# Fused attention and two MLPs: the first tile's layer 1 with its last block made for all 512 tokens at once, and the second product of probabilities and values issued one half block sooner

## The chip, the cores and the metric

The kernel runs on one core of one Trainium2 chip. The metric is the device time of the launch in microseconds. The kernel before takes 1432.98 us, the median of 3 runs (1432.86 to 1433.89).

## The reference

Attention over pooled keys and values, followed by two feed-forward layers, all in float32:

```
k_p = k.reshape(B, H, 72, 8, 64).mean(3);  v_p likewise        # 576 positions pooled by 8
attn = softmax(q @ k_p^T / 8);  x = attn @ v_p                 # B = H = 8, S = 576, D = 64
x = x as (4608 tokens, 512)
h = max(x @ w1, x @ w2, x @ w3);  x2 = h @ w_mid               # 512 -> 768 -> 512
y = x2 @ w_in;  out = (y - tanh(y)) @ w_out                    # 512 -> 2048 -> 512
```

## The kernel before, in words

**Tiling.** The 4608 tokens are 9 tiles of 512 (`TB`). Float32 products are made from operands split into a high and a low part, with three matmuls for each product (high by high, high by low, low by high; `split_passes`, line 611). Layer 1 of a tile is 6 blocks `m` of 128 hidden features. A block needs three products (w1, w2, w3; `NW`), each of 4 chunks `c` of the inputs and so of 12 matmuls: 36 matmuls in all. Attention comes in steps of 128 tokens: "score" (products of q and keys), "exp", "norm" (sums of rows and their inverse), "turn" (normalise, then transpose), and "attend", the product of probabilities and values, which gives `x`. The attends are listed in `ATTENDS` (line 84): two of 256 tokens for tile 0, then one of 512 for each tile.

**Order.** `make_order` (line 106) writes one list, `ORDER`. PE, DVE, ACT and SP each walk this list and do their share of every entry, so an entry's place sets the order on every queue at once. Within an entry the engines meet through semaphores. The entries are these:
- `("l1", t, m, lo, hi)` is block m of tile t for the tokens lo to hi. On PE it is `layer1` (line 672). On ACT it is `copy_first` (line 854), which copies the first product out of PSUM. On DVE it is `take_max` (line 1101): L1108 takes the maximum with the second product, L1113 that with the third.
- `("h1", ...)` splits this maximum: ACT makes the high part (L866), DVE the low part (L1119), which raises `h1_ready`.
- `("score", n)` is L625 on PE, then L1057 and L1061 on DVE and L847 on ACT. `norm` is L1073, L1076 and L1079, `turn` is L1087 and L1092, all on DVE.
- `("attend", n)` is L665 on PE, L852 on ACT and L1098 on DVE. The last of these raises `x_ready`.
- `("high", i)` splits a piece of weights on ACT (L837). For `w123` blocks 2 to 5 and both halves of `w_mid` POOL makes the low part (L590).
- `kred` and `vred` pool the keys and values of a batch on DVE (L1040, L1047). They stand in a list `waiting`, and each `fill()` puts the next group of it into the order.
- `("l2", t, c)` is a 512-token block of the middle layer, 18 matmuls on PE (L696), three for each m. For c = 0 PE waits before each m until `h1` of that block is ready. DVE takes it apart in `x2_sums` (line 1122).

**Tile 0.** Each of the 6 blocks is made twice: for tokens 0 to 255 as soon as the first attend has given them, and for tokens 256 to 511 after the second attend. There are thus 12 entries of 36 matmuls of 256 columns. Score 4 and 5 follow the first block of the second half, score 6 and 7 the fourth.

**PSUM.** Banks 0 to 3 are shared out by a counter (lines 183 to 190): each l1 entry takes the next three banks in turn, each l2 entry the next one, modulo 4. PE's `open_bank` (line 630) waits until the bank's use before has been drained. There are 60 l1 entries and 36 l2 entries, 216 uses in all. The last four are the l2 blocks of the last tile in the order c = 0, 2, 1, 3; they fall on banks 0, 1, 2, 3. The last of them is drained in DVE's step 2 at L1144, the one before it at L1142.

**The seam to the last layers.** After step 2 of the 72 steps of the large layer, PE runs `first_project`, the first products with `w_out`, which accumulate in banks 0 to 3 for the four groups j of 128 tokens. `project` (line 706) waits, for m = 0, until bank j has been drained of all its uses:

```python
                    for js in ((0, 1), (2, 3)):
                        for c in range(2):
                            project(c, js)
...
                    if m == 0:
                        if t == 0:
                            pe.wait_ge(drained[j], BANK_USES[j])
```

DVE's step 2 has, between the two halves of its own work, the two lines

```python
                    x2_sums(("l2", NT - 1, C_ORDER[2]))
                    x2_sums(("l2", NT - 1, C_ORDER[3]))
```

Of the kernel before, what the change touches and what calls it, by code (L numbers as in the profile page):

```python
# [22 lines left out]
MC1 = FF1 // P  # L23
# [4 lines left out]
TB = 512  # L28
NT = TOKENS // TB
SUB = TB // P  # L30
HALF = TB // 2
# [26 lines left out]
UNITS = STEPS2 * KHALF  # L58
# [28 lines left out]
def products_until(t, pair=PAIRS - 1):  # L87

    return PAIRS * (t + 1) + pair + 1
# [16 lines left out]
def make_order():  # L106

    o = [("kred", 0, p) for p in range(PAIRS)] + [
        ("warm", 14), ("score", 0), ("score", 1), ("exp", 0), ("exp", 1), ("warm", 14), ("pool_v",), ("warm", 6), ("norm", 0),
        ("high", 0), ("norm", 1), ("turn", 1), ("turn", 0), ("low", 0), ("attend", 0), ("high", 1), ("low", 1), ("high", 2)]  # L110
    waiting = []

    def then(*entries):
        for e in entries:
            o.append(e)
            if e[0] == "score" and e[1] != 3:
                o.append(("exp", e[1]))
            if e[0] == "score" and e[1] in LAST_STEP[:-2]:
                b = LAST_STEP.index(e[1]) + 2
                waiting.extend([[("kred", b, 0), ("kred", b, 1)], [("kred", b, 2), ("kred", b, 3)]])  # L120
            if e[0] == "attend" and 2 <= e[1] < B:
                waiting.extend([[("vred", e[1], 0), ("vred", e[1], 1)], [("vred", e[1], 2)]])

    def fill():
        if waiting:
            o.extend(waiting.pop(0))

    def l1(t, m, lo, hi):
        then(("l1", t, m, lo, hi), ("h1", t, m, lo, hi))

    def split(*pieces):
        return [(part, i) for i in pieces for part in ("high", "low")]

    waiting.extend([[("kred", 1, 0), ("kred", 1, 1)], [("kred", 1, 2), ("kred", 1, 3)],
                    [("vred", 1, 0)], [("vred", 1, 1)], [("vred", 1, 2)]])
    after_l1 = [[("high", 3), ("score", 2), ("score", 3), ("norm", 2), ("turn", 2)], [("high", 4), ("norm", 3)],
                [("high", 5), ("turn", 3)], [("high", 6)], [("attend", 1)], [("high", 7)]]
    for m in range(MC1):
        if m == 1:
            then(("l1", 0, m, 0, HALF), ("exp", 3), ("h1", 0, m, 0, HALF))  # L140
        else:
            l1(0, m, 0, HALF)
        then(*after_l1[m])
        if m > 1:
            fill()

    for t in range(NT):
        a = 4 * t + 4
        after_l1 = [[("score", a), ("score", a + 1), ("norm", a), ("turn", a)], [("norm", a + 1), ("turn", a + 1)], [],
                    [("score", a + 2), ("score", a + 3), ("norm", a + 2), ("turn", a + 2)],  # L150
                    [("norm", a + 3), ("turn", a + 3)], []]
        if t == 0:
            after_l1[4:] = [[], [("norm", a + 3), ("turn", a + 3)]]
        if t == NT - 1:
            after_l1 = [[("load", ("out", 0))], [("load", ("out", 1)), ("load_w", 0)], split(8) + [("load_w", 1)], split(9),
                        [("load_x2",)], []]
        for m in range(MC1):
            l1(t, m, HALF if t == 0 else 0, TB)
            if t > 0 and MC1 * (t - 1) + m < 2 * UNITS:
                then(("w_split", (MC1 * (t - 1) + m) // 2, m % 2))  # L160
            then(*after_l1[m])
            if m in (2, 4, 5):
                fill()
        if t == NT - 1:
            break
        for i, c in enumerate(C_ORDER):
            then(("l2", t, c))
            if i % 2:
                then(("x2_split", t, i // 2))
            if i == 1:  # L170
                then(("attend", t + 2))
            if i % 2:
                fill()

    then(("l2", NT - 1, C_ORDER[0]), ("step", 0), ("x2_part", NT - 1, C_ORDER[1]), ("step", 1),
         ("step", 2), ("first_project",))
    assert not waiting
    return o


ORDER = make_order()

USES, BANK_USES, _at = {}, [0] * 4, 0
for _e in ORDER + [("l2", NT - 1, c) for c in C_ORDER[1:]]:
    if _e[0] in ("l1", "l2"):
        USES[_e] = []
        for _i in range(NW if _e[0] == "l1" else 1):
            USES[_e].append((_at % 4, BANK_USES[_at % 4]))
            BANK_USES[_at % 4] += 1
            _at += 1  # L190
L1_NUMBER = {e: i for i, e in enumerate(e for e in ORDER if e[0] == "l1")}
for _kind, _count in (("score", STEPS), ("exp", STEPS), ("norm", STEPS), ("turn", STEPS), ("attend", len(ATTENDS)), ("step", EARLY)):
    assert sorted(e[1] for e in ORDER if e[0] == _kind) == list(range(_count))
assert [e[1] for e in ORDER if e[0] == "high"] == list(range(len(PIECES) - len(LATE)))
# [2 lines left out]
def fused_attention_mlps(nc, q, k, v_0, v, w123_in, w_mid, w_in, w_out, out):  # L197
# [5 lines left out]
    with ExitStack() as ctx:  # L203
        def sem(name):
            return ctx.enter_context(nc.semaphore(name))
# [124 lines left out]
        h1_ready = sem("h1_ready")  # L330
# [46 lines left out]
        def wait_piece(eng, kind, n):  # L377
            if (kind, n) in LOW_ON_POOL:
                eng.wait_ge(low_by_pool, LOW_ON_POOL.index((kind, n)) + 1)
            else:  # L380
                eng.wait_ge(low_by_dve, LOW_ON_DVE.index((kind, n)) + 1)
# [228 lines left out]
        def _(pe):  # L610
            def split_passes():
                return ((0, 0), (0, 1), (1, 0))
# [17 lines left out]
            def open_bank(entry, n=0):  # L630
                bank, before = USES[entry][n]
                if before > 0:
                    pe.wait_ge(drained[bank], before)
                return bank
# [37 lines left out]
            def layer1(entry):  # L672
                _, t, m, lo, hi = entry
                if t == 0 and lo == 0:
                    wait_piece(pe, "w123", m)
                for n in range(NW):
                    bank = open_bank(entry, n)
                    for c in range(KC1):
                        if m == 0 and n == 0:
                            pe.wait_ge(x_ready, c + 1 if hi == HALF else products_until(t, c))  # L680
                        for ws, xs in split_passes():
                            mm = pe.matmul(psum[:, bank, 0:hi - lo], w123[:, m, ws, n, c, :],  # L682
                                           x[:, xs, c, lo:hi],
                                           start=(c == 0 and ws + xs == 0), stop=(c == KC1 - 1 and ws == 1))
                    mm.then_inc(filled[bank], 1)

            def layer2(entry, ms=range(MC1)):
                _, t, c = entry
                if t == 0 and c == 0:
                    wait_piece(pe, "mid", 1)  # L690
                bank = open_bank(entry)
                for m in ms:
                    if c == 0:
                        pe.wait_ge(h1_ready, L1_NUMBER[("l1", t, m, HALF if t == 0 else 0, TB)] + 1)
                    for ws, xs in split_passes():
                        mm = pe.matmul(psum[:, bank, :], w_mid_s[:, ws, m, c * P:(c + 1) * P], h1[:, xs, m, :],  # L696
                                       start=(m == 0 and ws + xs == 0), stop=(m == MC1 - 1 and ws == 1))
                if ms[-1] == MC1 - 1:
                    mm.then_inc(filled[bank], 1)
# [133 lines left out]
        def _(act):  # L833
# [20 lines left out]
            def copy_first(entry):  # L854
                i = L1_NUMBER[entry]
                _, t, m, lo, hi = entry
                bank = wait_filled(act, entry)
                nc.scalar.activation(first_copy[:, i % 2, 0:hi - lo], psum[:, bank, 0:hi - lo], ACT.Copy)\
                    .then_inc(drained[bank], 1)

            def h1_high(entry):
                i = L1_NUMBER[entry]
                _, t, m, lo, hi = entry
                bank, before = USES[entry][2]
                act.wait_ge(drained[bank], before + 1)
                nc.scalar.activation(h1[:, 0, m, lo:hi], best[:, i % 2, 0:hi - lo], ACT.Copy).then_inc(h1_hi_ready, 1)  # L866
# [162 lines left out]
        def _(dve):  # L1029
# [71 lines left out]
            def take_max(entry):  # L1101
                i = L1_NUMBER[entry]
                _, t, m, lo, hi = entry
# [11 lines left out]
            def h1_low(entry):  # L1115
                i = L1_NUMBER[entry]
                _, t, m, lo, hi = entry
                dve.wait_ge(h1_hi_ready, i + 1)
                nc.vector.tensor_tensor(h1[:, 1, m, lo:hi], best[:, i % 2, 0:hi - lo], as_f32(h1[:, 0, m, lo:hi]),  # L1119
                                        ALU.subtract).then_inc(h1_ready, 1)  # L1120
# [204 lines left out]
```

## Time and profile before

| | |
|---|---|
| Median of 3 runs | 1432.98 us |
| Profiled execution | 1433.14 us, its span 1431.3 us |
| PE busy | 1421.7 us, 99% of the span |
| DVE busy | 1015.7 us, 71% |
| ACT busy | 661.2 us, 46% |
| POOL busy | 97.0 us, 7% |
| DMA | 269.74 MB, mean 188 GB/s |
| Mean granted TensorE clock | 1.000 |

The span runs from the first to the last instruction. The 1.84 us by which the execution is longer lie around it. PE's busy time counts modelled ends of pipelined matmuls, so 99% says that it seldom waits, and not that it is at its peak. Matmuls and weight loads are each recorded with a line of the kernel; the helpers' lines are those named above.

### The profile page before, as it was taken

To read this page: it belongs to the slowest core of one execution; us is meant where nothing else is said; L and a number is where in the kernel's file an instruction comes from. 1 tells how busy PE (TensorE), PEld (TensorE's weight loads), DVE (VectorE), ACT (ScalarE), POOL (GpSimd) and SP (SyncE) were. 2 spreads that over 40 slices of the span, in tenths; PEclk is the share of its full clock that TensorE was granted. 3 is DMA by queue.
4 is the path that set the end of the run, shared out by engine and by line. 5 is a ranking of instruction groups with operands and counts; after the bars stand their busy time and mean duration, and the time that the engine had idled before them with its cause. 6 is when DMAs were issued, how large, how long until landed. Compare 5 with 4: busy or idle time off the path is not lost.

```text
span 1431.3 us, 26330 instructions
## 1 busy us (share of the span) xinstructions
PE 1421.7 (99%) x10788; PEld 1236.2 (86%) x10788; DVE 1015.7 (71%) x1764; ACT 661.2 (46%) x1291; POOL 97.0 (7%) x141
## 2 busy tenths in 40 slices
PE   8999999999999999999999999999999999999998
PEld 7988888888888878788889999899999999999897
DVE  7876666666666655534887777877777777777787
ACT  4322222222222221223666666666666666666655
POOL 3402121212121100000000000000000000000000
PEclk9999999999999999999999999999999999999999
DMA  9254444443534211155976665666756666575641
GB/s 345 82 184 139 165 140 165 142 163 125 185 121 157 86 71 41 66 185 194 371 258 243 228 249 210 233 235 220 259 213 247 217 226 252 204 274 201 212 177 52
DMA packets 81335, 269.74 MB, mean 188 GB/s; under 512 B 7168, under 2 KB 21504, under 8 KB 69568
## 3 DMA queue, kind: packets, MB, share of 16 engines
q1 hardware_dynamic: 81216, 268.07, 52.1%
q8 instruction: 85, 1.39, 0.4%
q14 instruction: 34, 0.28, 0.1%
HBM read 210.89 MB, written 57.15 MB: 187 GB/s over the span
## 4 chain that ended last, share of the span: by engine, by line
PE 98%; DMA 1%; DVE 1%; ACT 0%; issue 0%; SPq 0%; ACTq 0%
PE psum L682 31%; PE psum L722 27%; PE psum L744 25%; PE psum L696 10%; PE psum L625 2%; PE psum L665 2%; DMA v_first<-in_v 0%; DMA k_first<-in_k 0%; PE psum L817 0%; ACT g L897 0%; PE psum L644 0%; DVE w L1052 0%; DVE poly L1175 0%; DVE g L1154 0%; ACT w L837 0%
## 5 line engine op out<-in xcount | busy, mean ns | idle before, releaser
L682 PE MATMUL psum<-x,w 128*128 128x512 f32 (+1 forms) x2160 | 451.6, 369 | 2.5 <-issue 1.2
L682 PEld LDWEIGHTS psum<-x,w 128*128 128x128 f32 x2160 | 375.5, 188 | 72.9 <-issue 2.1
L722 PE MATMUL psum<-w_out_s,g 128*128 128x512 f32 x1668 | 391.7, 390 | 0.1
L722 PEld LDWEIGHTS psum<-w_out_s,g 128*128 128x128 f32 x1668 | 308.6, 188 | 61.6 <-DVE g L1154 0.5
L744 PEld LDWEIGHTS psum<-x_even,ring 128*128 128x128 f32 x1680 | 208.2, 192 | 3.4
L744 PE MATMUL psum<-x_even,ring 128*128 128x256 f32 x1680 | 210.3, 283 | 0.0
L913 ACT ACTIVATE copies<-psum 128x256 f32<-128x256 f32 x288 | 108.0, 381 | 219.3 <-PE psum L744 217.9
L744 PEld LDWEIGHTS psum<-x_odd,ring 128*128 128x128 f32 x1344 | 166.3, 192 | 2.5
L744 PE MATMUL psum<-x_odd,ring 128*128 128x256 f32 x1344 | 168.2, 283 | 0.0
L866 ACT ACTIVATE h<-best 128x512 fp32r<-128x512 f32 (+1 forms) x60 | 35.3, 589 | 276.7 <-DVE best L1113 276.7
L696 PE MATMUL psum<-h,w_mid_s 128*128 128x512 f32 x648 | 151.7, 391 | 0.0
L696 PEld LDWEIGHTS psum<-h,w_mid_s 128*128 128x128 f32 x648 | 120.7, 188 | 28.6 <-issue 3.4
L1154 DVE TENSOR_TENSOR g<-poly,g 128x512 fp32r<-128x512 f32 x140 | 96.5, 689 | 52.0 <-ACT g L897 51.9
L1159 DVE SCALAR_TENSOR_TENSOR poly<-poly,u_sq 128x512 f32<-128x512 f32 x144 | 98.6, 685 | 21.7 <-ACT poly L910 21.6
L897 ACT ACTIVATE g<-poly 128x512 fp32r<-128x512 f32 x140 | 89.0, 636 | 52.6 <-DVE poly L1175 46.8
L910 ACT ACTIVATE poly<-u_sq,shift_col 128x512 f32<-128x512 f32 x144 | 103.3, 718 | 2.4
L1175 DVE COPY_PREDICATED poly<-is_big,h 128x512 f32<-128x512 uint8 x136 | 100.6, 740 | 2.4
L1169 DVE SCALAR_TENSOR_TENSOR poly<-poly,h 128x512 f32<-128x512 f32 x144 | 98.6, 684 | 0.0
L1113 DVE TENSOR_TENSOR best<-psum,best 128x512 f32<-128x512 f32 (+1 forms) x60 | 38.3, 639 | 83.8 <-PE psum L682 83.0
L1171 DVE TENSOR_TENSOR h<-h,tanh_h 128x512 f32<-128x512 f32 x136 | 93.2, 685 | 0.0
L901 ACT ACTIVATE u_sq<-h 128x512 f32<-128x512 f32 x144 | 90.4, 628 | 3.5 <-DVE h L1191 1.3
L904 ACT ACTIVATE tanh_h<-h 128x512 f32<-128x512 f32 x136 | 84.3, 620 | 0.0
(84 smaller groups left out, 1026.2 us busy)
## 6 DMA issues: line engine op xcount, KB each, us to landing
ring<-w_scratch SPq DMA_DIRECT2D x72, 1024.0 KB, 7.3
ring<-w_scratch SPq DMA_DIRECT2D x72, 768.0 KB, 4.4
x_scratch<-x_stage SPq DMA_DIRECT2D x18, 1024.0 KB, 4.2
x_odd<-x_scratch SPq DMA_DIRECT2D x28, 512.0 KB, 5.6
x_even<-x_scratch SPq DMA_DIRECT2D x28, 512.0 KB, 5.5
x_scratch<-x_stage SPq DMA_DIRECT2D x18, 768.0 KB, 3.3
w_scratch<-w_stage SPq DMA_DIRECT2D x32, 384.0 KB, 2.6
v_raw<-in_v SPq DMA_DIRECT2D x21, 512.0 KB, 4.4
```

What stands on the lines that cost most here:

```text
L682: mm = pe.matmul(psum[:, bank, 0:hi - lo], w123[:, m, ws, n, c, :], x[:, xs, c, lo:hi], start=(c == 0 and ws + xs == 0), stop=(c == KC1 - ...
L696: mm = pe.matmul(psum[:, bank, :], w_mid_s[:, ws, m, c * P:(c + 1) * P], h1[:, xs, m, :], start=(m == 0 and ws + xs == 0), stop=(m == MC1 ...
L722: mm = pe.matmul(psum[:, j, :], g_of(c)[:, gs, j * P:(j + 1) * P], w_out_s[:, row_of(c), ws, :], start=(m == 0 and gs + ws == 0), stop=(m ...
L744: mm = pe.matmul(psum[:, bank, 0:HALF], ring[:, p % 2, n, j, ws], x2[t % 2][:, j, X_OF[n], xs], start=(fresh and j + ws + xs == 0), stop=( ...
L901: nc.scalar.activation(u_sq[:, e], h2[:, s % 2, e], ACT.Square).then_inc(sq_done, 1)
L910: nc.scalar.activation(poly[:, into], u_sq[:, e], ACT.Square, bias=shift_col[:, 0:1]).then_inc(sq_done, 1)
L913: nc.scalar.activation(copies[:, n], psum[:, main_banks(s)[1 if n == 3 else 0], 0:HALF], ACT.Copy)\
L1154: nc.vector.tensor_tensor(g_of(c)[:, 1, :], poly[:, e], as_f32(g_of(c)[:, 0, :]), ALU.subtract).then_inc(g_ready, 1)
L1159: nc.vector.scalar_tensor_tensor(out=poly[:, into], in0=poly[:, into], scalar=OFFSET, in1=u_sq[:, e], op0=ALU.add, op1=ALU.mult).then_inc( ...
L1169: nc.vector.scalar_tensor_tensor(out=poly[:, into], in0=poly[:, into], scalar=C2, in1=h, op0=ALU.mult, op1=ALU.mult)
L1171: nc.vector.tensor_tensor(h, h, gelu_of(s)[0][:, e], ALU.subtract).then_inc(dve_step, 1)
L1175: nc.vector.copy_predicated(poly[:, into], gelu_of(s)[1][:, e], h2[:, s % 2, e]).then_inc(h_drained, 1)
```

## The change

The first half of tile 0 (tokens 0 to 255) now has blocks 0 to 4 alone. Turn 3 comes after block 1 and not after block 2. The second attend comes after block 3 and not after block 4. Block 5 is then made once, for all 512 tokens, and waits for `x` of the second attend. After it come score 4 and 5 with norm 4 and turn 4, and one `fill()`. Blocks 0 to 4 of the second half follow, with score 6 and 7 after block 2, and `fill()` after blocks 1, 3 and 4. Tile 0 has 11 l1 entries where it had 12. The loop over tiles skips layer 1 for tile 0. `L1_LAST` holds the last entry of each block, for the middle layer's waits. The later tiles' entries are unchanged.

```diff
--- before.py
+++ after.py
@@ -133,9 +133,10 @@
 
     waiting.extend([[("kred", 1, 0), ("kred", 1, 1)], [("kred", 1, 2), ("kred", 1, 3)],
                     [("vred", 1, 0)], [("vred", 1, 1)], [("vred", 1, 2)]])
-    after_l1 = [[("high", 3), ("score", 2), ("score", 3), ("norm", 2), ("turn", 2)], [("high", 4), ("norm", 3)],
-                [("high", 5), ("turn", 3)], [("high", 6)], [("attend", 1)], [("high", 7)]]
-    for m in range(MC1):
+    after_l1 = [[("high", 3), ("score", 2), ("score", 3), ("norm", 2), ("turn", 2)], [("high", 4), ("norm", 3), ("turn", 3)],
+                [("high", 5)], [("high", 6), ("attend", 1)], [("high", 7)]]
+
+    for m in range(MC1 - 1):
         if m == 1:
             then(("l1", 0, m, 0, HALF), ("exp", 3), ("h1", 0, m, 0, HALF))
         else:
@@ -143,20 +144,27 @@
         then(*after_l1[m])
         if m > 1:
             fill()
+    l1(0, MC1 - 1, 0, TB)
+    then(("score", 4), ("score", 5), ("norm", 4), ("turn", 4))
+    fill()
+    after_l1 = [[("norm", 5), ("turn", 5)], [], [("score", 6), ("score", 7), ("norm", 6), ("turn", 6)], [], [("norm", 7), ("turn", 7)]]
+    for m in range(MC1 - 1):
+        l1(0, m, HALF, TB)
+        then(*after_l1[m])
+        if m in (1, 3, 4):
+            fill()
 
     for t in range(NT):
         a = 4 * t + 4
         after_l1 = [[("score", a), ("score", a + 1), ("norm", a), ("turn", a)], [("norm", a + 1), ("turn", a + 1)], [],
                     [("score", a + 2), ("score", a + 3), ("norm", a + 2), ("turn", a + 2)],
                     [("norm", a + 3), ("turn", a + 3)], []]
-        if t == 0:
-            after_l1[4:] = [[], [("norm", a + 3), ("turn", a + 3)]]
         if t == NT - 1:
             after_l1 = [[("load", ("out", 0))], [("load", ("out", 1)), ("load_w", 0)], split(8) + [("load_w", 1)], split(9),
                         [("load_x2",)], []]
-        for m in range(MC1):
-            l1(t, m, HALF if t == 0 else 0, TB)
-            if t > 0 and MC1 * (t - 1) + m < 2 * UNITS:
+        for m in range(MC1 if t > 0 else 0):
+            l1(t, m, 0, TB)
+            if MC1 * (t - 1) + m < 2 * UNITS:
                 then(("w_split", (MC1 * (t - 1) + m) // 2, m % 2))
             then(*after_l1[m])
             if m in (2, 4, 5):
@@ -189,6 +197,8 @@
             BANK_USES[_at % 4] += 1
             _at += 1
 L1_NUMBER = {e: i for i, e in enumerate(e for e in ORDER if e[0] == "l1")}
+
+L1_LAST = {e[1:3]: e for e in ORDER if e[0] == "l1"}
 for _kind, _count in (("score", STEPS), ("exp", STEPS), ("norm", STEPS), ("turn", STEPS), ("attend", len(ATTENDS)), ("step", EARLY)):
     assert sorted(e[1] for e in ORDER if e[0] == _kind) == list(range(_count))
 assert [e[1] for e in ORDER if e[0] == "high"] == list(range(len(PIECES) - len(LATE)))
@@ -676,7 +686,7 @@
                 for n in range(NW):
                     bank = open_bank(entry, n)
                     for c in range(KC1):
-                        if m == 0 and n == 0:
+                        if n == 0 and (m == 0 or (t, m, lo, hi) == (0, MC1 - 1, 0, TB)):
                             pe.wait_ge(x_ready, c + 1 if hi == HALF else products_until(t, c))
                         for ws, xs in split_passes():
                             mm = pe.matmul(psum[:, bank, 0:hi - lo], w123[:, m, ws, n, c, :],
@@ -691,7 +701,7 @@
                 bank = open_bank(entry)
                 for m in ms:
                     if c == 0:
-                        pe.wait_ge(h1_ready, L1_NUMBER[("l1", t, m, HALF if t == 0 else 0, TB)] + 1)
+                        pe.wait_ge(h1_ready, L1_NUMBER[L1_LAST[t, m]] + 1)
                     for ws, xs in split_passes():
                         mm = pe.matmul(psum[:, bank, :], w_mid_s[:, ws, m, c * P:(c + 1) * P], h1[:, xs, m, :],
                                        start=(m == 0 and ws + xs == 0), stop=(m == MC1 - 1 and ws == 1))
```

## Rows read from the trace of the kernel before

Times are in us from the span's start unless marked ns. A row of an engine in order of time has its start, its length, the engine, line and operation, output and input with their shapes, and in brackets how long the engine was idle before it and who ended that.

**Rows 1.** The page: the chain that ended last, by engine, and the granted clock in 40 slices.
```profile
PEclk9999999999999999999999999999999999999999
...
PE 98%; DMA 1%; DVE 1%; ACT 0%; issue 0%; SPq 0%; ACTq 0%
```

**Rows 2.** The chain in order of time, around tile 0: start us, us, what.
```profile
30.37 14.29 PE psum L682 x117
...
46.14 8.82 PE psum L682 x72
54.97 1.64 PE psum L625 x103
...
80.53 8.20 PE psum L696 x36
...
100.11 8.21 PE psum L682 x36
```

**Rows 3.** DVE in order of time, tile 1: start us, us, engine, line, operation, idle before.
```profile
108.36 0.69 DVE L1113 TENSOR_TENSOR best<-psum,best 128x512 f32<-128x512 f32 x1 [1.56 <-PE psum L682]
...
110.35 0.75 DVE L1057 TENSOR_REDUCE row_max<-psum 128x8 f32<-128x576 f32 x1
```

**Rows 4.** DVE in order of time, tile 0's second half.
```profile
56.99 0.75 DVE L1057 TENSOR_REDUCE row_max<-psum 128x8 f32<-128x576 f32 x1
...
62.97 0.38 DVE L1108 TENSOR_TENSOR best<-psum,first_copy 128x256 f32<-128x256 f32 x1
...
64.70 0.75 DVE L1073 TENSOR_REDUCE row_sum<-probs 128x8 f32<-128x576 f32 x1
...
67.62 0.39 DVE L1108 TENSOR_TENSOR best<-psum,first_copy 128x256 f32<-128x256 f32 x1
...
69.36 1.21 DVE L1047 TENSOR_REDUCE v_pooled<-v_raw 128x128 f32<-128x1024 f32 x1
70.49 0.41 DVE L1108 TENSOR_TENSOR best<-psum,first_copy 128x256 f32<-128x256 f32 x1
...
72.26 0.75 DVE L1057 TENSOR_REDUCE row_max<-psum 128x8 f32<-128x576 f32 x1
...
78.24 0.38 DVE L1108 TENSOR_TENSOR best<-psum,first_copy 128x256 f32<-128x256 f32 x1
...
79.98 1.41 DVE L1040 TENSOR_REDUCE k_pooled<-k_raw 128x72 f32<-128x576 f32 x2
81.30 0.42 DVE L1108 TENSOR_TENSOR best<-psum,first_copy 128x256 f32<-128x256 f32 x1
...
82.73 0.42 DVE L1119 TENSOR_TENSOR h<-best,h 128x256 fp32r<-128x256 f32 x1 [0.48 <-ACT h L866]
```

**Rows 5.** DVE in order of time, tile 0's first half.
```profile
35.05 0.20 DVE L1079 RECIPROCAL row_inv<-row_eps 128x8 f32<-128x8 f32 x1
...
37.91 1.85 DVE L1087 TENSOR_TENSOR probs<-probs,row_inv 128x576 f32<-128x576 f32 x1
...
47.56 1.41 DVE L1098 TENSOR_TENSOR x<-psum,x 128x256 fp32r<-128x256 f32 x4
```

**Rows 6.** Line L1087: count, duration ns min/median/max, first and last start.
```profile
L1087 DVE TENSOR_TENSOR probs<-probs,row_inv x35: 757/759/1848, 13.9 to 580.7; 128x576 f32<-128x576 f32 x35
```

**Rows 7.** POOL in order of time, the low parts of blocks 4 and 5.
```profile
35.15 8.29 POOL L590 TENSOR_TENSOR w<-w_raw,w 128x512 fp32r<-128x512 f32 x6 [4.82 <-ACT w L837]
```

**Rows 8.** PE in order of time, the first products with w_out.
```profile
684.76 5.63 PE L722 MATMUL psum<-w_out_s,early_g 128*128 128x512 f32 x24
```

**Rows 9.** DVE in order of time, beside it.
```profile
686.75 0.42 DVE L1144 TENSOR_TENSOR x_stage_raw<-psum,x_stage_raw 128x256 f32<-128x256 f32 x1
```

**Rows 10.** The chain at PE's first wait for x: start us, us, what.
```profile
19.36 0.14 issue
```

**Rows 11.** PE in order of time, two stretches of warm-up matmuls of one shape.
```profile
1.10 5.40 PE L704 MATMUL psum<-ones 128*128 128x128 f32 x28 [1.10 <-POOL ones L570]
...
9.11 3.39 PE L704 MATMUL psum<-ones 128*128 128x128 f32 x28
```

## The prediction, made before the kernel was built

> **What bounds the kernel now.** I read the chain that ended last first: 98% of it is PE, and the granted clock is full in every slice [rows 1]. A change pays only if it shortens PE's own work, and costs whatever it makes PE wait. Next I read the chain in order of time around tile 0, because it gives the price of a block of each width and shows no gap between 30.37 us and the middle layer [rows 2]. Since PE is gapless there, what matters is how close the other engines are behind it. So I read DVE in order of time: in the second half of tile 0 it runs from 56.99 to 83.15 us with hardly a pause [rows 4]. Last I went to a place far away, where PE starts on w_out, because the bank of every later PSUM use hangs on the number of l1 entries [rows 8, 9].
>
> **PE's own work.** Removed: two passes over block 5 of 36 matmuls each at 256 columns; added: one of 36 at 512 columns. Two half blocks took 8.82 us, the whole block in tile 1 took 8.21 us [rows 2]. The gain is 0.61 us. The rest of PE's work (scores, attend, the ten other half blocks) only changes places.
> The isolated gap of the Trainium skill ("TensorE: Matmul & The Clock Gate", Back-to-back issue gap) has a fixed part of 2.5 ns for each matmul, which would make this an estimated 36 x 2.5 ns = 0.09 us. The two rows differ by 17 ns for each matmul saved, and they decide.
>
> **The second attend, one half block sooner.** Old PE times first: 117 matmuls from 30.37 took 14.29 us, 0.122 each, and the attend stood at 44.66, with 1.48 us to 46.14 [rows 2]. With 36 matmuls fewer ahead of it, it stands at 40.26 and ends at 41.74. It needs turn 3, which DVE now does right after norm 3, from about 35.3 us [rows 5]. The normalising multiply usually takes 0.76 us [rows 6]. Old turn 3 took 1.85 [rows 5] while POOL was at work [rows 7], and POOL starts on block 4 at 35.15, so I take 1.85. The transpose is then over at about 38.1, two microseconds ahead of the attend. Behind turn 3 on DVE waits `take_max` of block 2, now at 38.1 to 38.5. PE wants its bank for the third product of block 3 at 30.37 + 69 x 0.122 = 38.8. That is free by 0.3 us; a second delay of 1.1 us by POOL would turn it into a stall of 0.8 us, and the multiply at its usual 0.76 us leaves 1.4 us. ACT's split of the weights of block 5 follows `h1` of block 2 and so moves to about 39.4 to 40.9; POOL's three subtractions (half of 8.29 us, [rows 7]) end at about 45.0. PE needs them at 46.15, so the margin is 1.1 us. The split of `x` on DVE took 1.41 us [rows 5] and has PE's half block 4 (4.41 us) as its cover, as it had half block 5 before; ahead of it stands a weight split of ACT, and I get the last `x` at 46.1 to 46.4, where the first product needs only chunk 0 and chunk 3 comes 2 us later. Cost of this part: nothing, bounds 0 and +1 us. On SP, the loads of queries, keys and values keep their partners, and all these are used more than 10 us after issue: nothing. The wait for `x` inserted in `layer1` has behind it on PE block 5, and nothing else that could run.
>
> **DVE behind the whole block.** New times on PE: half block 4 ends at 46.15, block 5 at 54.36, the scores (1.64 us) at 56.00, which is 0.61 sooner than before. In tile 1 the whole block ended at 100.11 + 8.21 = 108.32 [rows 2] and DVE reached the scores at 110.35 [rows 3], 2.03 us later. So DVE starts on score 4 at 56.39. From there every entry is queued without a pause. The durations are differences of starts in [rows 4]: score 4 and 5 with norm and turn 4, 5.98 (56.99 to 62.97); vred, 1.13 (69.36 to 70.49), **which now stands here**, while before it stood ahead of the scores, where DVE had time; maximum and split of half block 0, 1.73; norm 5 and turn 5, 2.92; half block 1, 1.74; the last vred, 1.13; half block 2, 1.77; score 6 and 7 with norm and turn 6, 5.98; half block 3, 1.74; two kred, 1.32; half block 4 to the end of its low part, 1.85 (81.30 to 82.73 + 0.42). The sum is 27.29 us, and the last low part is ready at 83.68; with 0.14 us from DVE to PE [rows 10] PE can go on at 83.82.
> PE without stalls would begin the middle layer at 80.53 - 0.61 = 79.92. Before, the last block to be ready was block 5, which PE needs after 15 matmuls. Now it is block 4, needed after 12: 12 x 8.20/36 = 2.73 us, at 82.65 [rows 2]. By ends of matmuls the wait is 1.17 us. By starts, which lie 0.16 sooner, it is 1.33. I take **+1.25 us**. It will show in pieces, since DVE also frees banks late: I expect the first and largest (0.7 us) at the third product of half block 1, which waits for L1108 of half block 0. Smaller ones follow at half blocks 2 and 4 and before m = 4 of the middle layer. The old margin at the end was 80.53 + 15 x 0.228 - 83.15 = 0.8 us; it goes for 1.13 (vred) and 0.68 (three matmuls sooner) and little else. Bounds: +0.5 if DVE gains on these durations, +2 if POOL disturbs it.
>
> **The banks.** One l1 entry fewer is 3 uses fewer: 213 in place of 216. The last four uses, of the last tile's middle layer, fall on banks 1, 2, 3, 0 where they fell on 0, 1, 2, 3. The last of them, drained last by DVE at L1144, is now in bank 0. `first_project` begins with j = 0, so its very first matmul waits for L1144, which ended at 686.75 + 0.42 = 687.17 [rows 9]. PE arrived at 684.76 [rows 8]. Before, the banks that were drained last belonged to j = 2 and 3, reached only after 12 of the 24 matmuls that take 5.63 us [rows 8], at 687.5, and that hid all of it. Now PE resumes at 687.17 + 0.14 = 687.31. The price is 2.55 us by starts, and 2.4 if the 0.16 us overlap with the matmuls before is taken off: **+2.5 us**. Nothing that DVE or ACT does up to there depends on where PE then stands, so they can't come sooner; the wait has the whole large layer behind it, and that is PE alone to the end, so it isn't given back. Every other use of banks 0 to 3 is rotated together with its predecessor and costs nothing.
>
> **Sum.** -0.61 + 1.25 + 2.5 = +3.1 us on the profiled execution's 1433.14 (span 1431.3 and 1.84 around it), 1436.3. The median of the runs is 0.16 lower: **1436.1 us**, +0.22%.
>
> **Rivals.**
> 1. **The bank stall doesn't come** (the count of uses misread, or DVE frees bank 0 in time). For it: the code's waits on banks look alike, and the trace has no wait there. Against: DVE's queue at 686.75 [rows 9]. Then 1433.0 - 0.6 + 1.25 = 1433.6. Chance 0.07.
> 2. **DVE keeps up in tile 0**, and only the bank stall counts: the chain is 27.3 us against 82.65 - 56.39 = 26.3 of PE, so a gain of DVE of 4 to 5% is enough. 1433.0 - 0.6 + 2.5 = 1434.9; with half of the delay, 1435.5. Chance 0.18.
> 3. **Neither**: only the saved matmuls are seen, and the kernel ends faster or level, 1432.4. This is the other side. Its place is the same two waits. It decides from the point where L1144 ends before PE's last product of step 2, 2.4 us sooner than [rows 9] has it. Chance 0.03.
> 4. **The first half stalls too**: POOL holds DVE a second time at turn 3, or block 5's low weights come after 46.15. Up to 1 us more for either, 1437 to 1438. Chance 0.1.
> 5. **PE's pause costs clock.** PE's idle 2.5 us could let the granted clock fall from 2.4 to 1.2 GHz. The first 28 warm-up matmuls took 5.40 us, the next 28 took 3.39 [rows 11]: such a restart costs about 2.0 us more, 1438.1. Against it: granted clock full in every slice [rows 1], though PE had pauses of over 1 us. Chance 0.02.
> The same page of the Trainium skill (What's actually happening) says that PE's clock is halved when PE has been idle for a while and that activity restores it; by that rule rival 5 gives 1438.1, and no slice of this trace shows such a fall.
>
> **How the numbers follow.** The forecast with both stalls has 0.6 and spreads over 1435.4 to 1437.0. A measurement of this kernel can tell about 0.2%, 2.9 us, from no change; the line lies at 1435.85. Of the 0.6, 0.46 lie above it and 0.14 below; with rivals 4 and 5 (0.12) that is 0.58 slower. Within 0.2%: 0.14 and nearly all of rivals 1 to 3, 0.40. Faster by 0.2% would need a gain of 2.9 us, and PE's work gives 0.6: 0.02. For the range I leave out rivals 1, 3 and 5 and half of 4 and take 1434.5 to 1437.5.
>
> **What the changed profile would show.** Right: the attend near 40.3 us; 36 matmuls of 512 columns in 8.2 us from about 46.1 without a wait; DVE's vred right behind turn 4; PE waits on DVE L1108 after 60 us and on L1119 in the middle layer, together some 1.2 us; PE idle for 2.3 to 2.5 us ahead of L722, ended by DVE L1144. Wrong: no wait at L722 (my count of banks), a wait at the whole block for x or for POOL's weights (my reading of the first half), or a span that moves by less than either stall because something later had slack that the chain doesn't show.

## The result and the profile after

The changed kernel takes 1438.68 us (median of 7 runs, 1437.08 to 1439.32), the kernel before beside it 1433.57 (1432.86 to 1435.0). The ratio is 1.0036, 95% interval 1.0026 to 1.0045: slower by 5.1 us. In five later runs beside fifteen of the kernel before it was 1439.34 against 1433.88, ratio 1.0041 (1.0028 to 1.0054). The forecast was 1436.1 with a range up to 1437.5. The direction was right, and the time lies outside the range. In this document "clock" beside a run's time is the mean granted TensorE clock of the whole execution, in which 3.4 us at half speed show as about 0.999.

The profiled execution took 1438.68 us. First the page's lines that answer to those of before:

```profile
span 1436.8 us, 26251 instructions
...
PEclk9999999999999999999999999999999999999999
...
PE 95%; DVE 4%; ACT 1%; issue 1%; DMA 0%; SPq 0%; DVEq 0%; ACTq 0%
```

Each digit of `PEclk` covers a slice of 36 us. The chain is no longer PE alone: 4% of it is DVE. Where, the chain in order of time shows (start us, us, what), here around tile 0:

```profile
28.62 0.94 issue
29.55 8.53 PE psum L692 x69
38.08 0.02 issue
38.10 1.69 PE psum L692 x12
39.80 1.48 PE psum L675 x48
41.28 12.71 PE psum L692 x72
53.99 0.02 issue
54.01 0.70 DVE best L1123
```

Against [rows 2]: the second attend stands at 39.80 and block 5, now made whole, needs no wait of its own (72 matmuls, half of them of 512 columns, in 12.71 us; forecast 12.62). At 38.10 PE starts again behind a short wait, in which a bank came free from DVE (L1118, which is L1108 of before). Then DVE takes over the chain. Its queue in order of time (start, length, line, operation, idle before):

```profile
37.66 0.39 DVE L1118 TENSOR_TENSOR best<-psum,first_copy 128x256 f32<-128x256 f32 x1
...
56.01 0.75 DVE L1067 TENSOR_REDUCE row_max<-psum 128x8 f32<-128x576 f32 x1
...
61.98 1.18 DVE L1057 TENSOR_REDUCE v_pooled<-v_raw 128x128 f32<-128x1024 f32 x1
63.08 0.41 DVE L1118 TENSOR_TENSOR best<-psum,first_copy 128x256 f32<-128x256 f32 x1
...
64.84 0.74 DVE L1083 TENSOR_REDUCE row_sum<-probs 128x8 f32<-128x576 f32 x1
...
67.76 0.39 DVE L1118 TENSOR_TENSOR best<-psum,first_copy 128x256 f32<-128x256 f32 x1
...
69.50 1.21 DVE L1057 TENSOR_REDUCE v_pooled<-v_raw 128x128 f32<-128x1024 f32 x1
70.63 0.41 DVE L1118 TENSOR_TENSOR best<-psum,first_copy 128x256 f32<-128x256 f32 x1
...
72.40 0.75 DVE L1067 TENSOR_REDUCE row_max<-psum 128x8 f32<-128x576 f32 x1
...
78.36 0.39 DVE L1118 TENSOR_TENSOR best<-psum,first_copy 128x256 f32<-128x256 f32 x1
...
82.86 0.42 DVE L1129 TENSOR_TENSOR h<-best,h 128x256 fp32r<-128x256 f32 x1 [0.48 <-ACT h L876]
```

This answers to [rows 4]. From score 4 at 56.01 to the low part of the last half block, 82.86 + 0.42 = 83.28, are 27.27 us; the forecast had 27.29, entry by entry. The vred at 61.98 stands between turn 4 and the first maximum. PE in order of time shows what waits for it, and then the seam:

```profile
55.49 7.46 PE L692 MATMUL psum<-x,w 128*128 128x256 f32 x60
63.54 6.35 PE L692 MATMUL psum<-x,w 128*128 128x256 f32 x48 [0.59 <-DVE best L1118]
...
80.34 8.77 PE L706 MATMUL psum<-h,w_mid_s 128*128 128x512 f32 x36
```

```profile
654.69 4.28 PE L706 MATMUL psum<-h,w_mid_s 128*128 128x512 f32 x18
659.11 3.18 PE L754 MATMUL psum<-x_even,ring 128*128 128x256 f32 x24
...
684.56 1.59 PE L754 MATMUL psum<-x_even,ring 128*128 128x256 f32 x12
688.55 7.32 PE L732 MATMUL psum<-w_out_s,early_g 128*128 128x512 f32 x24 [2.40 <-DVE x_stage_raw L1154]
```

PE idles 0.59 us for L1118 at 63.54, and the middle layer's first 36 matmuls take 8.77 us. Against [rows 8] the first products with w_out start at 688.55, after PE was idle for 2.40 us, and DVE's L1154 (L1144 of before, [rows 9]) releases them:

```profile
687.98 0.42 DVE L1154 TENSOR_TENSOR x_stage_raw<-psum,x_stage_raw 128x256 f32<-128x256 f32 x1
```

Up to here this is the forecast. But the 24 matmuls then take 7.32 us and not 5.63. The view of stretches of time (stretch, us, PE busy and matmuls, granted clock, DMA share, GB/s) says why:

```profile
686.00:688.50 2.50, 0.15 (x2) 1.00 1.02 431
688.50:690.00 1.50, 1.45 (x5) 0.68 0.98 382
690.00:692.00 2.00, 2.00 (x6) 0.50 1.05 387
692.00:694.00 2.00, 2.00 (x9) 0.89 1.06 388
694.00:696.00 2.00, 2.00 (x12) 1.00 0.86 314
```

Some 0.5 us after PE had started again the granted clock fell to 0.50, the level of 1.2 GHz. It stayed there for 3.4 us and then was 1.00 (2.4 GHz) again. The page's line `PEclk` reads 9 in all 40 slices even so: in a slice of 36 us, a fall of 3.4 us doesn't show.

**Where the 5.5 us of span went**, between the two profiled executions: from PE's first long run of layer 1 (30.37 before, 29.55 after) to the end of those 24 matmuls (690.39, 695.87) it took 6.3 us more. Block 5: -0.61. First half of tile 0: +0.36 (81 matmuls in 10.25 us against 81 x 0.122 = 9.89). From there to the third attend: +1.44 (47.83 us; before 42.59, to which 3.80 of work were added). From there to the seam: +0.48 in this execution, pieces of up to 0.15 us in the later tiles' scores. The seam's first matmuls: +0.37. The bank wait: +2.56, the 2.40 of idle time and the 0.16 by which the first of the 24 matmuls overlapped the matmuls before it when there was no wait. The clock: +1.69 (7.32 against 5.63). Ahead of 29.55 the first loads landed 0.8 us sooner by chance, and behind 696 nothing changed.

### The profile page after: what moved, and what is told of

Read it like the earlier page. It is cut to its first block, busy times and chain, and to the rows that moved or that the text cites. A ratio compares the mean times of both kernels' runs of the same rounds, so it can differ in the third digit from the quotient of the medians.

```text
span 1436.8 us, 26251 instructions
## 1 busy us (share of the span) xinstructions
PE 1425.2 (99%) x10752; PEld 1235.9 (86%) x10752; DVE 1014.4 (71%) x1761; ACT 661.1 (46%) x1289; POOL 96.4 (7%) x141
## 4 chain that ended last, share of the span: by engine, by line
PE 95%; DVE 4%; ACT 1%; issue 1%; DMA 0%; SPq 0%; DVEq 0%; ACTq 0%
PE psum L692 30%; PE psum L732 27%; PE psum L754 25%; PE psum L706 10%; PE psum L675 2%; PE psum L635 2%; DVE probs L1071 0%; DVE row_max L1067 0%; DMA k_first<-in_k 0%; DVE poly L1185 0%; DVE row_sum L1083 0%; DVE poly L1179 0%; DVE probs L1097 0%; PE psum L827 0%; DVE h L1181 0%
```

## The experiments

### 1. The banks' order, and the queue of DVE

`e1_banks` takes the late bank last:

```diff
-                    for js in ((0, 1), (2, 3)):
+                    for js in ((1, 2), (3, 0)):
```

> The changed kernel, with first_project taking the groups j in the order (1, 2), (3, 0) and not (0, 1), (2, 3), so that the bank drained last comes last again. Theory A (the wait for bank 0 lasts 2.4 us, and the halved clock behind it costs 1.85 us more): both go, 4.2 us less than the changed kernel, the launch about 1434.5 us or 1.0 us above the kernel before, granted clock 1.000, and the 24 matmuls of the first products with w_out take 5.6 us and not 7.3. Rival B (the slow 24 matmuls come from DMA traffic or from what they read, not from the pause): only 2.4 us go, about 1436.3. Rival C (some later wait takes the place of this one): less than 2 us go.

Measured: 1435.33 us against 1433.10, ratio 1.0016 (1.0007 to 1.0025): 2.2 us above the kernel before, where the changed kernel is 5.1 to 5.5 above it. PE's row at the seam:

```profile
686.56 5.63 PE L732 MATMUL psum<-w_out_s,early_g 128*128 128x512 f32 x24
```

No pause, 5.63 us, granted clock 1.00. Theory A holds for the mechanism, and B and C fall; the launch is 0.8 us above what A expected. (The texts of what was expected put the clock at 1.85 us. That counts in the 0.16 us of overlap; the rows give 1.6 to 1.7.) In the trace, from PE's first long run to here, the kernel is 1.22 us slower than before, as A has it (655.61 us against 654.39). The rest lies ahead of it, in the landing of the first loads, and is taken up below.

`e4_vred` adds to this the move of one `fill()`:

```diff
         if m > 1:
             fill()
+        if m == MC1 - 2:
+            fill()
     l1(0, MC1 - 1, 0, TB)
     then(("score", 4), ("score", 5), ("norm", 4), ("turn", 4))
-    fill()
```

> As e1_banks, and one pooling of values (vred 1, 1) is put on DVE ahead of the whole block 5, where DVE waits for PE, instead of behind turn 4. Theory A (DVE's queue from score 4 to the middle layer is what PE waits for in tile 0, 27.3 us without a pause): the queue is 1.13 us shorter, PE's waits in tile 0's second half shrink from some 1.4 to 0.3 us, and the launch is 1.1 us below e1_banks, about 1433.4, level with the kernel before. Rival B (PE waits there for single banks that don't follow from the length of the queue): less than 0.4 us below e1_banks.

Measured: 1434.05 us, 1.28 below `e1_banks`; ratio to before 1.0006 (0.9997 to 1.0015). The wait at L1118 is gone: three half blocks run through.

```profile
56.00 13.28 PE L693 MATMUL psum<-x,w 128*128 128x256 f32 x108
...
79.74 8.73 PE L707 MATMUL psum<-h,w_mid_s 128*128 128x512 f32 x36
```

So the length of DVE's queue was the cause, and the 1.13 us of vred were the most of it. The second row keeps a rest, 8.73 us for 36 matmuls that took 8.36 before.

`e8_combo` adds the other term, the three matmuls by which PE had come to need the last block sooner:

```diff
-                for m in ms:
+                for m in ((0, 1, 2, 3, 5, 4) if (t, c) == (0, 0) else ms):
...
-start=(m == 0 and ws + xs == 0), stop=(m == MC1 - 1 and ws == 1))
+start=(m == 0 and ws + xs == 0),
+stop=(m == (4 if (t, c) == (0, 0) else MC1 - 1) and ws == 1))
```

> e4_vred, and the first product of the middle layer of tile 0 takes block 5 ahead of block 4, so that PE needs the last finished block after 15 matmuls again and not after 12. Theory A (what is left of the wait in tile 0, 0.37 us, is DVE's queue against those three matmuls): the middle layer's first 36 matmuls take 8.4 us as before and not 8.7, the launch is 0.4 us below e4_vred, at 1433.6. Rival B (another wait stands right behind it): no change.

Measured: 1433.66 us against 1433.11, ratio 1.0006 (0.9998 to 1.0015), 0.39 below `e4_vred`; that difference of medians alone would prove little, but the row shows it:

```profile
79.76 8.36 PE L707 MATMUL psum<-h,w_mid_s 128*128 128x512 f32 x36
```

8.36 us as before. From PE's first long run to the second tile (30.33 to 99.35) this kernel takes 69.02 us, the kernel before 69.58 (30.37 to 99.95): with both waits away, the 0.6 us of block 5 are there.

### 2. The bank wait without the new layer 1

`e2_stall_only` is the kernel before with this alone:

```diff
-                    for js in ((0, 1), (2, 3)):
+                    for js in ((3, 0), (1, 2)):
```

> The kernel before, with only first_project's order changed to (3, 0), (1, 2), so that it begins with the bank that is drained last; layer 1 is untouched. Theory A: the bank wait alone, with the clock behind it, costs 4.2 us, about 1437.8, with PE idle for 2.4 us ahead of the first products with w_out and a granted clock near 0.5 for 3 to 4 us after it. Rival B (the clock falls only together with something in the new layer 1 order): 2.4 us, about 1436.0, clock 1.000. Rival C (the bank wait is hidden here): 1433.6.

Measured: 1437.54 us against 1433.10, ratio 1.003 (1.0019 to 1.0042), clock 0.998 or 0.999 in all six runs. So 4.4 us go on this edit alone.

```profile
682.44 1.59 PE L744 MATMUL psum<-x_even,ring 128*128 128x256 f32 x12
686.44 7.28 PE L722 MATMUL psum<-w_out_s,early_g 128*128 128x512 f32 x24 [2.41 <-DVE x_stage_raw L1144]
```

```profile
684.00:686.00 2.00, 0.03 (x1) 1.00 1.02 428
686.00:688.00 2.00, 1.56 (x4) 0.60 0.99 394
688.00:690.00 2.00, 2.00 (x7) 0.54 1.06 390
690.00:692.00 2.00, 2.00 (x11) 1.00 1.06 387
```

The same pause (2.41 us), the same fall, and 7.28 us for the 24 matmuls. Most of the change's loss needs nothing of the change but its three uses of banks fewer.

`e6_half_stall` is the kernel before with the order `((2, 3), (0, 1))`, which shortens the pause:

> The kernel before, with first_project's order changed to (2, 3), (0, 1): it begins with the bank drained by L1142, 0.45 us ahead of L1144. Theory A: PE pauses 2.0 us in place of 2.4 (and 0.7 us later bank 3 is free, without a wait), so the pause costs 2.0 to 2.1 us; whether the clock falls behind a pause of this length is what the run shows: 1435.2 without the fall, 1437.0 with it. Rival B (the price of a pause at this place doesn't follow its length): as e2_stall_only, 1437.5.

Measured: 1437.31 us against 1433.88 (11 runs), ratio 1.0021 (1.0012 to 1.003), 3.4 us above the kernel before where `e2_stall_only` was 4.4. The profiled one has a pause of 1.96 us, released by L1142, and a fallen clock. Of the 11 runs, 7 had a granted clock of 0.999 and a median of 1437.48; 4 had 1.000 and 1436.1. This suggests that a pause of the same length at the same place takes the clock down in some executions and leaves it in others, with a difference of 1.4 us; the mean clock doesn't say where a fall was, and two traces below show it. The expected 1435.2 for the second kind was 0.9 too low.

### 3. Is it the pause that takes the clock down?

`e3_warm` fills the pause of the changed kernel with work that is thrown away:

```diff
+                    pe.wait_ge(drained[1], BANK_USES[1])
+                    for _ in range(18):
+                        pe.matmul(psum[:, 1, 0:P], ones[:], ones[:], start=True, stop=True)
                     for js in ((0, 1), (2, 3)):
```

> The changed kernel, with 18 small matmuls of 128 columns on a tile of ones, put into bank 1 right before the wait for bank 0, where PE would be idle (18 x 0.12 = 2.2 us, inside the pause of 2.4). Their results are overwritten. Theory A (the pause takes the clock down): the clock stays at 1.000 and the 24 matmuls behind take 5.6 us; 1.85 us less than the changed kernel where its clock had fallen, about 1436.8. Rival B (the clock falls for another reason, such as the products before it): no change, 1438.7.

Measured: 1439.25 us, clock 1.000 in all five runs. I had counted wrong: each such matmul is recorded as two, so this was 4.18 us of filler in a pause of 2.4. The time says nothing, the rows do:

```profile
686.24 4.18 PE L816 MATMUL psum<-ones 128*128 128x128 f32 x36
690.18 5.73 PE L732 MATMUL psum<-w_out_s,early_g 128*128 128x512 f32 x24
```

No pause, no fall, 5.73 us. `e7_warm9` has half the filler:

> The changed kernel, with 9 matmuls on ones (18 recorded, 18 x 0.11 = 2.0 us) in PE's pause ahead of the first products with w_out; e3_warm had twice that, 4.0 us, and so put 1.5 us of its own on top. Theory A (the pause of 2.4 us takes the clock down and that costs 1.85 us): clock 1.000, PE reaches the first products at the same distance behind L1154 as in the changed kernel, the 24 matmuls take 5.6 us, launch about 1437.0, 1.7 us below the changed kernel's 1438.7. Rival B (the clock's fall is worth less than the profile shows): within 0.5 us of the changed kernel.

Measured: 1437.94 us (5 runs, 1437.14 to 1440.16), between the theories, so it was run again beside the changed kernel itself:

> The changed kernel again, unaltered, beside e11 on one chip, because e7_warm9 had five runs on another chip than the changed kernel's and its median, 1437.94, lies between the two theories. Expected: 1438.3 to 1438.9, granted clock 0.998 to 0.999 in most runs; runs with clock 1.000 about 1.4 us below the others.

> e7_warm9 again, unaltered. Theory A (the pause takes the clock down and that costs 1.7 to 1.85 us whenever it does): 1.2 to 1.8 us below e10_after_again. Rival B (the fall costs nothing that the launch feels): within 0.5 us of it.

Measured: 1439.34 us for the changed kernel, 1438.44 for the filled one. The difference of 0.9 us is less than A's 1.2 to 1.8 and more than B's 0.5, and by the launch alone neither is shown. Two things explain it in part. The changed kernel's clock doesn't fall in every run: its profiled execution here (`e10_after_again`) kept 1.00, with the pause in place:

```profile
690.33 5.68 PE L732 MATMUL psum<-w_out_s,early_g 128*128 128x512 f32 x24 [2.42 <-DVE x_stage_raw L1154]
```

```profile
690.00:692.00 2.00, 1.67 (x7) 1.00 0.96 381
```

And the filled kernel's clock can fall elsewhere, at the front, when the first loads come late and PE idles there (`e11_warm9_again`, pauses of 1.50 and 1.78 us before 10.41):

```profile
9.00:12.00 3.00, 1.59 (x69) 0.95 1.09 322
12.00:14.00 2.00, 2.00 (x12) 0.50 1.00 349
14.00:16.30 2.30, 2.30 (x19) 0.76 1.03 407
```

The seam of the filled kernel, in the same execution, kept its clock:

```profile
688.59 2.17 PE L816 MATMUL psum<-ones 128*128 128x128 f32 x18
691.17 5.68 PE L732 MATMUL psum<-w_out_s,early_g 128*128 128x512 f32 x24 [0.41 <-DVE x_stage_raw L1157]
```

The rows of the seam, from the end of the last 12 matmuls with `x_even` to the end of the 24, settle what the launches leave open: 9.72 us in the first trace of the changed kernel, where the clock fell, 8.10 in this one, where it didn't, and 8.09 with the filler. So the fall costs 1.6 us, and without a fall the seam takes as long with the filler as with the bare pause.

Over the twelve runs of the changed kernel, three had a granted clock of 1.000 (1437.08, 1437.65, 1438.69) and nine had 0.998 or 0.999 (1438.61 and more). Not each of the nine need be a fall at the seam: 5 of the 64 runs of the kernel before beside these experiments read 0.999 too. In all nine traces of kernels without this pause, or with it filled, the 24 matmuls took 5.63 to 5.73 us; in three of the four with a pause of 2.0 to 2.4 us they took 7.3. That the pause is what lets the clock fall is shown, by taking it away, by putting it into the kernel before and by filling it. That it does so each time is not so. What decides it from one execution to the next, no run shows.

### 4. The first half alone

`e5_attend_only` is the kernel before with turn 3 and the second attend sooner, block 5 in two halves:

```diff
-... [("high", 4), ("norm", 3)],
-                [("high", 5), ("turn", 3)], [("high", 6)], [("attend", 1)], [("high", 7)]]
+... [("high", 4), ("norm", 3), ("turn", 3)],
+                [("high", 5)], [("high", 6), ("attend", 1)], [("high", 7)], []]
```

> The kernel before, with only the second attend one half block sooner and turn 3 right behind norm 3; block 5 stays in two halves, all orders and banks of the later tiles stay. Theory A (turn 3, held up by POOL, delays the maximum of block 2, for whose bank PE waits at the third product of block 3): PE loses 0.2 to 0.4 us there and nothing elsewhere, the launch is 0.3 us above the kernel before, which a median of this kernel can't tell from nothing; the wait on L1108 near 38 us shows in the trace. Rival B (the sooner attend pays or costs more by moving other waits): over 1 us either way.

Measured: 1432.68 us against 1433.11, ratio 0.9999 (0.999 to 1.0007): no difference. PE took 9.97 us for the 81 matmuls ahead of the attend, 0.08 more than 81 x 0.122. The changed kernel and those made from it took 9.97 to 10.17 in seven traces, so the 10.24 of the profile after is the unlucky end of this.

### 5. The load ahead of the large layer

All kernels with the new order, up to the one below, showed PE some 0.2 to 0.6 us late at the first matmuls of step 0, and none with the old order did. They wait for `x_even`, 3584 KB from DRAM. The DMA view gives the time from issue to landing, first before and then after:

```profile
x_even<-x_scratch SPq DMA_DIRECT2D x1, 3584.0 KB, 11.4
```

```profile
x_even<-x_scratch SPq DMA_DIRECT2D x1, 3584.0 KB, 12.2
```

Inside this load of the changed kernel lies a packet of instructions (queue q8, 16 KB), here in the one microsecond from 654.71; before, no such packet fell into it:

```profile
q1 hardware_dynamic: 15, 0.43, 99.6%
q8 instruction: 1, 0.02, 6.0%
```

`e9_pad` adds to `e8_combo` 72 waits that are long fulfilled to PE's stream, behind the two stretches of 14 warm-up matmuls each:

```diff
                     keep_warm(entry[1])
+                    if entry[1] == 14:
+                        for _ in range(36):
+                            pe.wait_ge(ones_ready, 1)
```

> e8_combo with 72 waits that are already fulfilled put into PE's stream in its pauses ahead of score 0 and of the first sums of v, as many instructions as block 5 made once has removed (36 matmuls and 36 weight loads). Theory A (every kernel with the new order loads x_even for the large layer in 12.2 us and those with the old one in 11.4, because a 16 KB packet of PE's own instructions now falls into that load; the number of PE's instructions sets when): the packet moves out of the load, the load takes 11.4 to 11.5 us again, and PE's wait of 0.3 us ahead of the large layer goes. Rival B (the load is longer for the changed order of the work itself): 12.2 us as in e8_combo. The launch moves by 0.3 us at most, so the trace decides.

```profile
x_even<-x_scratch SPq DMA_DIRECT2D x1, 3584.0 KB, 11.0
```

Measured: 11.0 us to landing, no packet of queue q8 in the load (it came at 647, ahead of the issue at 648.19), no wait at step 0; the launch 1433.33, 0.33 below `e8_combo`, which alone would be noise. Theory A holds in this one trace: the eight traces with the packet in the load have 12.1 to 12.5 us, the five without it 11.0 to 11.5. That adding instructions to PE's stream moves the packet is what says that they are PE's; why one packet holds up the load by so much is not shown. The unexplained pause of PE near 29 us ("issue", 0.9 to 1.35 us in every trace) moved too: it came after 27 matmuls of block 1 in all others and after 9 here, so it too hangs on the count of PE's instructions. That this is PE waiting for code is an inference; no row names it.

## Why the prediction was wrong

**PE's own work**: right. 0.61 us, and `e8_combo` shows 0.56 where the waits are away.

**The first half**: right that turn 3 would be held up by POOL (1.76 us at 34.97), that the bank for block 3 would be close and that `x` and the weights of block 5 would be in time. The cost was put at nothing with +1 as bound; it was 0.1 to 0.36.

**DVE behind the whole block**: right in place, cause and size. The queue took 27.27 us (27.29), the first wait came at the third product of half block 1 at L1118 (0.59 us, forecast 0.7), PE lost 1.44 us up to the third attend (forecast 1.25 in all). `e4_vred` and `e8_combo` gave it back in the two pieces named, 1.13 and about 0.4.

**The banks**: right. The wait was 2.40 us, released by L1154, at the first matmul, and cost 2.56 with the lost overlap (forecast 2.4 to 2.55).

**The step that failed is rival 5**, "PE's pause costs clock". Its price was sized well: 2.0 us against the 1.6 to 1.7 of the rows. Its chance, 0.02, was wrong, and so it was left out of the range. The argument against it was that the clock had stayed full in every slice [rows 1] though PE had pauses of over 1 us. Both halves of it were weak. The longest such pause was 1.25 us, half of the one that I forecast myself, and so those rows said nothing about 2.5 us. And slices of 36 us can't show a fall of 3.4 us: the page after has one and reads 9 in all 40. The pace of the warm-up matmuls [rows 11] had shown a low level that the clock column of the trace before does not:

```profile
1.10:3.00 1.90, 1.90 (x9) 1.00 0.55 171
```

These are 4.7 matmuls in a microsecond where rows 11 have 8.3 later on. And the rule of the Trainium skill ("TensorE: Matmul & The Clock Gate", What's actually happening), that idleness halves the clock, was on the table with the right mechanism; the fall to 0.50 behind 2.40 us of idle time agrees with it, the trace of `e10_after_again` with its 2.42 us doesn't. The clock fell behind the pause in 9 of 12 runs of the changed kernel, if each run with a granted clock under 1.000 is counted so, and by the same count in 6 of 6 of `e2_stall_only`. With 1.7 us added, the forecast of 1436.1 becomes 1437.8, above its range and still 0.9 below the measured 1438.68; the rest is below.

**What was missed** besides: 0.37 us at `x_even` (experiment 5), which goes when as many instructions are put back as were removed, and the 0.48 us in the later tiles' scores (0.2 and 0.3 in `e8_combo` and `e1_banks`), whose cause was not looked for.

**What stays open**: 0.6 to 1.2 us. `e1_banks`, `e4_vred`, `e8_combo` and `e9_pad` are all that much above what their traces account for between layer 1's start and 690 us, and behind 690 us all kernels take the same (741.1 us). What is left is the front, where PE's long run of layer 1 began between 29.55 and 33.01 us in the eight traces of the new order without the added waits and between 29.95 and 30.66 in four of the old. In the late ones the first `q` or `k` landed late or the clock fell in the warm-up. Nothing in the order differs there, and no run was made that tells chance from cause.

No version beats the kernel before. `e5_attend_only` (1432.68) and `e9_pad` (1433.33) can't be told from it, and the most that block 5 can give is 0.6 us of 1433.

## What to carry to other kernels

Where PSUM banks are dealt out in turn by a counter, every entry added or removed turns the wheel for all later uses. Count its use number modulo the banks at each place that names banks by hand, above all at a seam: here three uses fewer, 600 us earlier, cost more than everything around the edited blocks. Price a forecast pause of PE twice, as the pause and as slow matmuls behind it, and take as evidence against the second only pauses of that length, read in stretches as short as the fall would be. And when a filler job of 1.1 us on a helping engine is moved, ask on which side of its idle time it ends up.

## What the runs showed of the hardware that was not expected

- Behind a pause of 2.0 to 2.4 us TensorE's granted clock fell to 0.50 (1.2 GHz) for some 3.4 us in three of four traces, which cost 1.6 to 1.7 us in the rows (24 matmuls in 7.28 to 7.32 us against 5.63 to 5.68) and 1.4 us between runs of one kernel. By the mean clock of the runs it stayed at 1.00 in 3 of 12 with the pause of 2.4 us, and in 4 of 11 with that of 1.96 us.
- Adding 72 instructions to PE's stream moved a 16 KB packet of code out of a 3.6 MB load (one trace). With such a packet inside, the load landed 0.6 to 1.5 us later than without (12.1 to 12.5 us in eight traces against 11.0 to 11.5 in five).
